# Products of 512 moving columns issued as two of 256 in the steady passes of the first network

## The reference, cut to what matters

```python
def _moe_ref(x, w_gate, w_val, w_out, rms_g):        # first network
    rms = np.sqrt(np.mean(x * x, axis=-1, keepdims=True) + 1e-06)
    xn = x / rms * rms_g
    g = xn @ w_gate
    silu = g * (1.0 / (1.0 + np.exp(-g)))
    val = xn @ w_val
    return (silu * val @ w_out).astype(np.float32)

def _moe2_ref(x, w1, w2, w3, w_out):                 # second network
    h = np.maximum(np.maximum(x @ w1, x @ w2), x @ w3)
    return (h @ w_out).astype(np.float32)
```

## Time and profile before

| | |
|---|---|
| median of 3 runs | 1063.11 us (1062.24 to 1064.55) |
| span of the profiled execution | 1055.6 us (its time outside the span is not on the page) |
| instructions in the page | 17238 |
| TensorE products, busy | 1010.7 us, x5760 |
| TensorE weight loads, busy | 884.7 us, x5760 |
| VectorE, busy | 630.4 us, x1083 |
| ScalarE, busy | 251.6 us, x500 |
| GpSimd, busy | 493.3 us, x548 |
| granted TensorE clock, mean | 0.989 |
| data moved | 64.56 MB, mean 61 GB/s |

### The profile page before, as it was taken

One profiled execution on the slowest core, in us unless ns is written; L12 is line 12 of the kernel. 1 busy time (PEld: TensorE's weight loads), 2 busy tenths in 40 slices (PEclk: granted clock), 3 DMA queues, 4 the chain that ended last, 5 costly groups with the idle time before them and its releaser, 6 DMA issues.

```text
span 1055.6 us, 17238 instructions
## 1 busy us (share of the span) xinstructions
PE 1010.7 (96%) x5760; PEld 884.7 (84%) x5760; DVE 630.4 (60%) x1083; ACT 251.6 (24%) x500; POOL 493.3 (47%) x548
## 2 busy tenths in 40 slices
PE   4778989899999999999999999999999999999998
PEld 4678988888888888888888888888788888888887
DVE  8978798987776877687787777444331312121221
ACT  1233312222122121312122212323331212121211
POOL 7655586767574756565756757121020201011111
PEclk9789999999999999999999999999999999999999
DMA  6533212303111221204030310211301010101000
GB/s 198 161 94 105 77 54 68 93 30 117 34 65 57 85 65 43 76 1 137 11 108 12 117 33 4 90 45 47 118 1 60 1 60 9 51 15 45 22 7 30
DMA packets 36216, 64.56 MB, mean 61 GB/s; under 512 B 4928, under 2 KB 22720, under 8 KB 36160
## 3 DMA queue, kind: packets, MB, share of 16 engines
q1 hardware_dynamic: 30288, 52.12, 15.4%
q10 hardware_dynamic: 5872, 11.80, 3.8%
HBM read 54.46 MB, written 9.44 MB: 61 GB/s over the span
## 4 chain that ended last, share of the span: by engine, by line
PE 84%; DVE 6%; POOL 5%; issue 3%; ACT 1%; DMA 0%; SPq 0%; POOLq 0%; DVEq 0%
PE ps_sc L477 9%; PE ps_acc L459 8%; PE ps_acc L461 8%; PE ps_acc L460 8%; PE ps_gate L459 6%; PE ps_val L459 5%; PE ps_val L461 5%; PE ps_gate L460 5%; PE ps_gate L461 5%; PE ps_val L460 5%; PE ps_desk L500 4%; PE ps_sc L460 2%; PE ps_sc L459 2%; PE ps_sc L461 2%; POOL kT L1119 2%
## 5 line engine op out<-in xcount | busy, mean ns | idle before, releaser
L477 PE MATMUL ps_sc<-rB,kT 128*128 128x128 f32 x1152 | 161.5, 287 | 25.8 <-DVE A L900 12.4
L477 PEld LDWEIGHTS ps_sc<-rB,kT 128*128 128x128 f32 x1152 | 154.9, 200 | 37.2 <-DVE rB L877 19.6
L1119 POOL TENSOR_TENSOR kT<-kT,wT 128x256 f32<-128x256 f32 x168 | 142.9, 851 | 86.0 <-PE ps_sc L477 58.1
L1184 POOL TENSOR_TENSOR h_lo<-h2f,h_hi 128x512 fp32r<-128x512 f32 x36 | 46.4, 1290 | 253.6 <-ACT h_hi L822 253.6
L1091 POOL TENSOR_TENSOR h_lo<-act_h,h_hi 128x512 fp32r<-128x512 f32 (+1 forms) x83 | 98.1, 1182 | 109.5 <-ACT h_hi L676 104.4
L1124 POOL TENSOR_TENSOR rB<-rB,wT 64x256 f32<-64x256 f32 x144 | 120.0, 833 | 11.3
L877 DVE TENSOR_TENSOR rB<-rB,wT 64x256 f32<-64x256 f32 x144 | 96.5, 675 | 37.8 <-PE ps_sc L477 28.4
L459 PE MATMUL ps_gate<-x_hi,wg_hi 128*128 128x512 f32 (+1 forms) x252 | 97.4, 386 | 7.7 <-DVE act_h L853 5.8
L676 ACT ACTIVATE h_hi<-act_h 128x512 fp32r<-128x512 f32 (+1 forms) x84 | 48.0, 571 | 227.9 <-DVE act_h L856 227.6
L900 DVE COPY_PREDICATED A<-mask,ps_sc 128x512 f32<-128x512 uint8 x120 | 98.7, 822 | 0.0
L672 ACT ACTIVATE act_h<-ps_gate 128x512 f32<-128x512 f32 (+1 forms) x84 | 45.0, 536 | 217.7 <-PE ps_gate L461 217.6
(11 more groups left out here) (135 smaller groups left out, 2071.8 us busy)
## 6 DMA issues: line engine op xcount, KB each, us to landing
kT<-in_k_channels SPq DMA_DIRECT2D x24, 256.0 KB, 3.5
wT<-in_w_channels SPq DMA_DIRECT2D x24, 256.0 KB, 4.0
rB<-in_r_channels SPq DMA_DIRECT2D x48, 128.0 KB, 2.7
kL<-in_k_tokens SPq DMA_DIRECT2D x24, 192.0 KB, 2.4
rL<-in_r_tokens SPq DMA_DIRECT2D x24, 192.0 KB, 2.5
vL<-in_v_tokens SPq DMA_DIRECT2D x24, 192.0 KB, 2.4
x_scratch<-x1s SPq DMA_DIRECT2D x6, 768.0 KB, 4.3
xn<-x_scratch SPq DMA_DIRECT2D x6, 768.0 KB, 4.3
```

What stands on the lines that cost most here:

```text
L477: last = mm(ps_sc[:, j, q * T:(q + 1) * T], kT[2 * duo + j][:, q, :], rights, start=True, stop=True)
L1119: tt(half(kT[b][:, :, :], h, 0), half(kT[b][:, :, :], h, 0), block_decay(b, h, 1), ALU.mult).then_inc(k_scaled, 1)
```

## The change

Where a part has more than 256 tokens, its products are made for the first half of the tokens and then for the second. In `gate_or_val` the halves are the outer loop and the chunks the inner; in `hidden_out` the blocks of output are the outer loop and the halves the inner. The flags that start and end a sum are set accordingly: in `gate_or_val` each half starts its own, in `hidden_out` only the first half of the first block does. Passes 0 and 1 keep their products. The semaphore is raised by the last product of a part, as before.

```diff
@@ -533,6 +533,13 @@
+            def halves(toks):
+
+                first, width = toks.start, toks.stop - toks.start
+                if width <= TOK // 2:
+                    return [toks]
+                return [slice(first, first + width // 2), slice(first + width // 2, toks.stop)]
+
             def gate_or_val(n, f, wt, bank, used, full):
@@ -541,10 +548,11 @@
                 after(pe, used, n, FC, f)
-                for c in range(KC):
-                    cols = slice(f * P, (f + 1) * P)
-                    last = split_products(bank[:, toks], (wt[0][:, c, cols], wt[1][:, c, cols]),
-                                          (x_hi[:, c, toks], x_lo[:, c, toks]), c == 0, c == KC - 1)
+                cols = slice(f * P, (f + 1) * P)
+                for part_of in halves(toks):
+                    for c in range(KC):
+                        last = split_products(bank[:, part_of], (wt[0][:, c, cols], wt[1][:, c, cols]),
+                                              (x_hi[:, c, part_of], x_lo[:, c, part_of]), c == 0, c == KC - 1)
                 last.then_inc(full, 1)
@@ -559,8 +567,12 @@
                 for d in range(KC):
                     cols = slice(d * P, (d + 1) * P)
-                    last = split_products(ps_acc[:, d, toks], (wo[0][:, f, cols], wo[1][:, f, cols]),
-                                          (h_hi[:, f % 2, toks], h_lo[:, f % 2, toks]), f == 0, f == FC - 1)
+                    for at, part_of in enumerate(halves(toks)):
+                        own = ps_acc[:, d, part_of]
+                        w_hi, w_lo = wo[0][:, f, cols], wo[1][:, f, cols]
+                        t_hi, t_lo = h_hi[:, f % 2, part_of], h_lo[:, f % 2, part_of]
+                        first, final = f == 0 and at == 0, f == FC - 1 and part_of.stop == toks.stop
+                        last = split_products(own, (w_hi, w_lo), (t_hi, t_lo), first, final)
                 last.then_inc(out_done, 1)
```

## The result

The changed kernel takes 1068.18 us (median of 4 runs) against 1062.67 (4 runs), a ratio of 1.0057 with a 95% interval of 1.003 to 1.0083: slower by 0.6%, 5.5 us between the medians and 6.1 by the ratio. Timed once more beside the experiments, with 11 runs, the ratio is 1.0063 (1.004 to 1.0085). 1070.9 was forecast.

What follows compares the result with a forecast made beforehand. TensorE's rate of starting instructions was taken as the bound from 217 to 748 us. Span 1055.6 + 1.2 (products) + 6.6 (three missed jumps) = 1063.4 us; median 1063.11 + 7.8 = 1070.9 us, range 1062.0 to 1077.0.

Steps and rivals of the forecast that it cites:

- case A: TensorE's loop over steady tiles: one instruction packet missed at each of three jumps; 1070.9 us, own range 1066 to 1077, chance 0.72.
- Products, +1.2 us: First network's split parts: 120 gate and val parts 0.02 us shorter, 60 out parts 0.06 longer; together +1.2 us.
- The miss, 2.2 us a jump: TensorE's jump back to the loop top: larger loop not held, a packet awaited; 2.2 us a jump, 6.6 in three.
- the pause: TensorE's jump back: VectorE's 2.7 us from branch to register operation, plus 0.8 for TensorE's longer packet.
- The cover: Products already queued on TensorE at the jump, running from 444.70 until gate starts at 446.91 us, hide part of the wait.
- a gap behind the branch: Sign at three jumps: 2.7 to 3.5 us instead of 0.1 between TensorE's branch and the register operation behind it.
- Refetching inside a turn at nothing: Instruction packets fetched within TensorE's loop turn cost nothing; if that fails, each of some 8 could cost up to 2 us.
- Case B: TensorE's larger loop still held, no pause at the jump, only +1.2 stays: 1064.3 us, at quickest just below 1063; chance 0.16.
- D: All split parts go at the quick distance of 0.114 us and nothing is missed: 1056.5 us; chance 0.03.
- C: A price per product: gate and val pay what out pays, no miss; +10.8 us, 1073.9 us; chance 0.04.
- E: TensorE's loop: two packets in series at a jump, or refetching not hidden inside the turn; +17 us, 1081.3 us; chance 0.05.
- The 7.5 us between span and median: Whole run: median 1063.11 us lies 7.5 above the 1055.6 span; carried over unchanged to the forecast.

## Why the prediction was right

The forecast, case A, came true in sign, place and size, and one packet is waited for at each jump, as it had assumed: +7.8 us forecast, +7.4 and +7.1 in the two profiles of the changed kernel over the stretch, 6.1 and 6.7 us by the ratios of the whole runs.

- **Products, +1.2 us.** Measured +1.7 written out against written out, or 4 x 0.4 in the last turns less 0.2 in pass 6. Out paid 0.08 a part instead of 0.06: the nine products of the earlier trace rows had not settled, and in 18 on end the distance goes to 120 ns, as the earlier trace rows showed behind an attention block. Gate and val gave 0.022 a part in the loop of the changed kernel, as forecast (0.0125 where out is whole), and 0.04 to 0.06 in its pass 6, where the distance goes to 113 ns and stays. By these, 48 x 0.08 - 96 x 0.022 = 1.7 in the loop and 12 x 0.08 - 12 x 0.04 - 12 x 0.06 = -0.2 in pass 6.
- **The fixed price of a product**, 2.5 ns by the Trainium skill (TensorE: Matmul & The Clock Gate, Back-to-back issue gap), would have been 4 us, an estimate by that page. The page gives it for a product on its own, which the prediction does not say; for a stream of weight loads and products it gives 131 ns at 512 columns. The trace shows neither: about 230 ns at 512 columns, which is no more than twice the 113 to 120 at 256.
- **The miss, 2.2 us a jump.** Measured 2.3, 2.0, 1.6 and, again, 1.7, 1.8, 1.9. Its terms, at the first jump: the pause was to be 2.7 + 0.8 = 3.5 us; the branch took 3.78 where it takes 0.22, so 3.6. The cover was to be 1.5 us; from the branch's normal end, 337.2 + 0.2, to the start that gate would have had, 339.24, it is 1.8. From the end of the branch to the first product: 341.36 - 340.98 = 0.4 us, forecast 0.2. 3.6 - 1.8 + 0.4 = 2.2. The 0.8 for a longer packet fits too: VectorE's pause in the earlier trace rows has the same three parts, 1.02 us to its packet, 0.35 for it and 1.42 behind it, while TensorE's packet takes 0.88 to 1.33. The branch varies, 3.3 to 3.8 us in this kernel, with when its packet starts and how long that takes; why a packet starts late is open.
- **Where it shows.** I had looked for a gap behind the branch, as VectorE has it. On TensorE it is the branch itself that lasts, 3.78 us, with the next instruction right behind it. Packets: 8 or 9 a turn were forecast, it is 8 and 2 more at the jump.
- **Refetching inside a turn at nothing:** right. In the last turn of the changed kernel and in the written-out one all code is fetched, and no product there waits for it.
- **Case B** (still held) was given 0.16 with an edge that no row showed. The edge is near 1700, so B was further off than I could know. Its own numbers do not agree: a quarter of B is counted as faster by more than 2.1 us, while its time is said to be just below 1063 at its quickest, and D with a quarter of B is 0.07, not 0.08. C, D and E did not come: the extra time of gate and val is negative, out never went at 114 ns, and there is no other wait in the loop.

Part of the agreement is luck: products were 0.5 us under, misses 0.7 to 1.2 over. Inside the miss the cover was 0.3 us longer than I had it, and the way from the branch to the first product 0.2 longer, which nearly cancel.

The 7.5 us between span and median were misread, without harm to the sum: they are not a fixed part of every execution. In the executions for which both numbers are known the time is 1.7 us above the span (1070.70 against 1069.0), so the profiled execution of the kernel before took some 1057.3 us, an estimate, and was a quick one.

## What to carry to other kernels

Splitting instructions in a loop has a price that no instruction shows: the loop's size on that engine. Count a turn's instructions, register and semaphore ones too, and look in the DMA view whether the engine's instruction packets stop after the first turn; if they do, there is something to lose, and here it was 2 us at each jump once a turn passed about 1700 instructions on TensorE. If a turn must be large, write the loop out: here the straight code was fetched without any wait, also at 2114 instructions a turn.

## What the runs showed that I had not expected

The edge: a loop of 1754 instructions is refetched in every turn, with 27 packets between 330 and 680 us, one of 1682 not at all. No middle ground was seen: a loop 4% larger than one that is held pays at every jump, as one of 2114 does.

And pass 6. In two of the 14 profiles it took 80.1 and 80.8 us instead of 75.6, with the loop itself undisturbed. ScalarE's timeline of the kernel with only out split, and what TensorE waited for:

```profile
683.13 0.35 ACTq L762 DMA_DIRECT2D stage<-in_moe_w  x1
...
683.51 1.79 ACTq L762 DMA_DIRECT2D stage<-in_moe_w  x1
...
685.33 2.23 ACTq L762 DMA_DIRECT2D xn<-in_moe_w  x2
687.94 0.60 ACT L684 ACTIVATE act_h<-ps_gate 128x512 f32<-128x512 f32 x1 [3.53 <-issue]
...
PE ps_gate L459 <- DVE act_h L865: 2.4, 1, 2.4
```

The issue of a DMA took 1.79 us, and two more 2.23 together, where such an issue takes 0.46 in each of the other twelve profiles; the sigmoid behind them came late, VectorE behind it, and TensorE stood 2.4 us for `ps_gate`. The stretches around it (columns as in the earlier trace rows, the granted clock third from the right):

```profile
680.60:686.60 6.00, 6.00 (x36) 5.14 (x34) 1.64 (x3) 2.27 (x5) 0.00 (x0) 1.00 0.41 142
686.60:692.90 6.30, 3.91 (x11) 2.80 (x10) 1.37 (x2) 1.23 (x2) 1.28 (x1) 0.75 0.71 243
```

The clock, 1.00 ahead of the wait, averages 0.75 in the stretch that holds the wait and the products behind it, so for a while behind the wait the products went at the lower of its two levels (1.2 GHz), 0.42 us from start to start where it is 0.23 otherwise:

```profile
690.80 0.63 PE L460 MATMUL ps_gate<-x_lo,wg_hi 128*128 128x512 f32 x1
691.22 0.63 PE L461 MATMUL ps_gate<-x_hi,wg_lo 128*128 128x512 f32 x1
```

The ten products from 689.31 to 693.28 us take 1.6 us more than ten at 0.23. With the wait of 2.4 and the 1.0 that the split out parts cost in pass 6, that makes 5.0 of the 5.2 us. The other profile that has it is of a kernel with a different loop; the twelve that do not have it include all four of the two kernels compared. What makes the issue slow I did not try.
